# One written list of places for attention, loads and weight pieces in a fused RWKV attention and two-MLP kernel

## The reference

```python
# attention, per batch and head, state is 48 x 48
for t in range(S):
    cur = einsum('bhd,bhe->bhde', u * kt, vt)
    y[t] = einsum('bhd,bhde->bhe', rt, state + cur)
    state = wt[..., None] * state + einsum('bhd,bhe->bhde', kt, vt)
x = y, heads side by side: (2, 768, 384)
# first MLP: 384 -> 1024, taps of 3 along the sequence, gate, -> 384
h = maximum(x @ w_in, 0)
x = (h * sigmoid(conv3(h, conv_w))) @ w_out
# second MLP: layer norm with g_ln, 384 -> 1536 -> 384, added to x
out = x + maximum(norm(x) * g_ln @ w_ch1, 0) @ w_ch2
```

## Time and profile before

| | |
|---|---|
| median of 3 runs | 433.77 us (432.04 to 434.29) |
| profiled execution | 434.07 us |
| its span, first to last instruction | 432.3 us |
| mean granted TensorE clock | 0.944 of full speed |
| TensorE busy | 373.3 us (86%) |
| VectorE busy | 243.1 us (56%) |
| ScalarE busy | 148.4 us (34%) |
| POOL busy | 87.3 us (20%) |

### The profile page before, as it was taken

How to read it: one execution, slowest core, us unless ns; L and a number is a source line. 1 busy time by engine, 2 the same in 40 slices (tenths; PEclk the granted TensorE clock), 3 DMA queues, 4 the chain that set the end, 5 groups by cost and what they waited for, 6 DMA issues and landing times.

```text
span 432.3 us, 8651 instructions
## 1 busy us (share of the span) xinstructions
PE 373.3 (86%) x3255; PEld 352.0 (81%) x3255; DVE 243.1 (56%) x498; ACT 148.4 (34%) x359; POOL 87.3 (20%) x150
## 2 busy tenths in 40 slices
PE   6669796779998499999789999699989699995995
PEld 5558695779998498999689998599988599994994
DVE  4565697795367773368763188862287721385120
ACT  1213384252256221256311256311256211463111
POOL 5344212240220411141032050032050000010001
PEclk9669989698999889999999999989999989998799
DMA  8489131556010133001321010301000000010001
GB/s 140 111 167 199 45 111 55 127 138 152 8 38 1 38 55 58 0 20 36 56 57 20 2 36 20 57 0 22 0 27 12 2 2 2 0 39 0 2 0 36
DMA packets 62786, 20.42 MB, mean 47 GB/s; under 512 B 56959, under 2 KB 61210, under 8 KB 62746
## 3 DMA queue, kind: packets, MB, share of 16 engines
q1 hardware_dynamic: 61520, 19.47, 20.5%
q10 hardware_dynamic: 1226, 0.41, 0.5%
HBM read 17.51 MB, written 2.36 MB: 46 GB/s over the span
## 4 chain that ended last, share of the span: by engine, by line
PE 46%; DVE 8%; ACT 4%; issue 3%; POOL 0%; POOLq 0%; DVEq 0%; ACTq 0%
PE hid L392 7%; PE acc L392 7%; PE hid L393 6%; PE hid L394 6%; PE acc L394 6%; PE acc L393 6%; ACT g_hi L638 2%; PE turn L1002 1%; DVE suf L826 1%; PE y_ps L1047 1%; PE y_ps L1055 1%; DVE g_lo L794 1%; DVE stats L927 1%; PE y_ps L1064 1%; PE pair_a L1020 1%
## 5 line engine op out<-in xcount | busy, mean ns | idle before, releaser
L951 DVE SCALAR_TENSOR_TENSOR g_lo<-hid,g_hi 128x256 fp32r<-128x256 f32 x72 | 30.3, 421 | 112.2 <-ACT g_hi L752 112.1
L752 ACT ACTIVATE g_hi<-hid 128x256 fp32r<-128x256 f32 x72 | 27.7, 385 | 157.2 <-PE acc L394 135.1
L392 PE MATMUL hid<-xc_hi,w_hi 128*128 128x256 f32 x216 | 66.7, 309 | 6.6 <-DVE xc_lo L941 4.9
L393 PE MATMUL hid<-xc_lo,w_hi 128*128 128x256 f32 x216 | 63.1, 292 | 0.0
L394 PE MATMUL hid<-xc_hi,w_lo 128*128 128x256 f32 x216 | 63.0, 292 | 0.0
L773 DVE SCALAR_TENSOR_TENSOR cg<-h_all,cols,cg 128x256 f32<-128x256 f32 x96 | 50.5, 526 | 6.0 <-ACT cg L706 5.4
L392 PEld LDWEIGHTS hid<-xc_hi,w_hi 128*128 128x128 f32 x216 | 43.0, 199 | 10.1 <-issue 6.1
L392 PE MATMUL acc<-w_hi,g_hi 128*128 128x384 f32 x144 | 49.0, 340 | 0.0
L394 PE MATMUL acc<-w_hi,g_lo 128*128 128x384 f32 x144 | 49.0, 340 | 0.0
L393 PE MATMUL acc<-w_lo,g_hi 128*128 128x384 f32 x144 | 48.7, 338 | 0.0
L392 PE MATMUL acc<-wout_hi,g_hi 128*128 128x384 f32 x96 | 35.1, 365 | 11.3 <-DVE g_lo L794 6.3
(11 more groups left out here) (143 smaller groups left out, 775.5 us busy)
## 6 DMA issues: line engine op xcount, KB each, us to landing
w_dec<-in_w SPq DMA_DIRECT2D x12, 192.0 KB, 3.8
k_in<-in_k SPq DMA_DIRECT2D x12, 192.0 KB, 4.3
out<-x SPq DMA_DIRECT2D x12, 192.0 KB, 1.9
r_in<-in_r SPq DMA_DIRECT2D x11, 192.0 KB, 4.0
raw<-in_moe_w_ch SPq DMA_DIRECT2D x4, 384.0 KB
v_in<-in_v SPq DMA_DIRECT2D x12, 96.0 KB, 2.7
cg<-in_moe_w_ch SPq DMA_DIRECT2D x3, 384.0 KB
h_all<-in_moe_w_ch SPq DMA_DIRECT2D x3, 384.0 KB
```

What stands on the lines that cost most here:

```text
L392: pe.matmul(out_ps, lh, rh, start=start and i == 0, stop=False)
L393: pe.matmul(out_ps, lh, rl, start=False, stop=False)
L752: act.activation(a_hi[j % 2][:, :], hid[j % 2][:, 0:GP], ACT.Relu)\
L951: dve.scalar_tensor_tensor(out=a_lo[j % 2][:, :], in0=hid[j % 2][:, 0:GP], scalar=0.0, in1=a_hi[j % 2][:, :].bitcast(F32), op0=ALU.max, op ...
```

## The change

One list of places, written by hand, takes the place of the generator for attention, and it holds loads and fetches too:

- FIRST is the opening. All loads of tiles 0 to 2 but v(2) are issued ahead of weights 0 to 2; six pieces of weights are made before the first hidden, the first of them behind x(1). The rest of the lists (GATING, NORM, TURN, SECOND_MLP) says per group which items follow which place. Hidden waits per j for its half of w_in: three pieces for j < 4, whose pieces now come by halves of the columns. w_in has its rows in plain order.
- A tile's work is cut finer: "scan1" (L811, L816) and "scan2" (the rest), "mid" (`k_mid` and `r_mid` together), "mask", "bonus", "state", "ruk", "middle" (v's middle columns to `v_mid`, POOL) are items of their own.
- k is transposed into `pair_a` and r into `pair_b`, and these wait for the mask of the tile before, not for `turn`; only w and ke use `turn`. In the opening kv uses `hid[1]`.
- `scores` and `bv` are doubled. The two score buffers serve as staging slots 4 and 5 from y(2) on. Pieces 4 to 13 go to `raw`, `x2` and the score buffers, from 14 on to `cg`, `h_all` and `raw`. All low parts are VectorE's.
- x windows: two instead of three; POOL writes the zero edges per tile.
- v comes in one load with the heads side by side, kv as eight matmuls (64 rows of output, 48 columns) instead of four, `bv` in one POOL operation instead of two.

In group 0's second MLP the list has tiles 3 and 4 whole, and tile 5 up to its mask. Between norm(g) and turn(g) stand w(3) | w(6), x(5) | w(9), x(7) | w(11), x(9) | x(11); behind turn(2) and turn(3) stand y(8) and y(10).

```diff
-    WSLOTS = SEQ // G
+    WSLOTS = 2
...
+                 *(t[:, :, :, :].rearrange("p a e s -> p (a e s)")[:, 0:PIECE] for t in scores)]
+        RAW, TWICE, LENT = 3, (1, 2), (4, 5)
...
-        EARLY, MIDDLE = 8, ch1 + half + 1
-        SLOT = ([i % NST for i in range(EARLY)] + [(0, NST - 1)[i % 2] for i in range(MIDDLE - EARLY)]
-                + [1 + i % (NST - 1) for i in range(NP - MIDDLE)])
-        ON_POOL = (1, 3, 5, *range(EARLY, ch1))
+        SECOND = ch1 + half + 1
+        SLOT = [1, 2, 3, 0, 3, 0, 4, 5, 3, 0, 4, 5, 3, 4] + [1 + i % 3 for i in range(NP - SECOND)]
+        ON_POOL = ()
...
-            last = {"in": N_IN - 1, "out": N_IN + j // 2,
+            last = {"in": (N_IN // 2 if j < JF // 2 else N_IN) - 1, "out": N_IN + j // 2,
...
+        FIRST = [("load_w", 0), ("load_k", 0), ("load_v", 0), ("load_w", 1), ("load_k", 1), ("load_r", 1),
+                 ("load_v", 1), ("w", 0), ("k", 0), ("r", 0), ("load_w", 2), ("ruk", 0), ("load_k", 2), ("load_r", 2),
+                 ("fetch", 0), ("fetch", 1), ("fetch", 2), ("middle", 0),
+                 ("scan1", 0), ("scan2", 0), ("w", 1), ("mid", 0), ("sc", 0), ("cols", 0), ("ke", 0),
+                 ("bonus", 0), ("scan1", 1), ("mask", 0), ("kv", 0), ("k", 1), ("r", 1), ("ruk", 1), ("scan2", 1),
+                 ("y", 0), ("w", 2), ("mid", 1), ("sc", 1), ("state", 0), ("x", 0), ("load_v", 2),
+                 ("middle", 1), ("fetch", 3), ("ke", 1), ("bonus", 1), ("scan1", 2), ("mask", 1), ("k", 2), ("r", 2),
+                 ("ruk", 2), ("kv", 1), ("scan2", 2), ("y", 1), ("middle", 2), ("state", 1), ("mid", 2), ("sc", 2),
+                 ("bonus", 2), ("x", 1), ("weights", 0), ("mask", 2), ("weights", 1), ("weights", 2), ("y", 2),
+                 ("weights", 3), ("x", 2), ("fetch", 4), ("fetch", 5), ("fetch", 6), ("fetch", 7),
+                 ("weights", 4), ("weights", 5),
+                 ("fetch", 8), ("fetch", 9), ("load_w", 3), ("load_k", 3), ("load_r", 3), ("load_v", 3)]
...
+        GATING[0] = {0: [("weights", 6), ("fetch", 10)], 1: [("weights", 7), ("fetch", 11)],
+                     2: [("weights", 8), ("fetch", 12)], 3: [("weights", 9), ("fetch", 13)],
+                     5: [("weights", 10), ("fetch", 16)],
+                     7: [("weights", 11)], 8: [("weights", 12), ("k", 3)], 9: [("r", 3), ("weights", 13)]}
+        NORM[0] = [("w", 3)]
+        TURN[0] = [("scan1", 3), ("fetch", 14), ("fetch", 15), ("load_w", 4), ("load_k", 4), ("load_r", 4), ("load_v", 4)]
+        SECOND_MLP[0] = {0: [("ke", 2), ("weights", 14), ("fetch", 17)],
+                         1: [("scan2", 3), ("ruk", 3), ("kv", 2), ("weights", 15), ("fetch", 18)],
+                         2: [("mid", 3), ("weights", 16), ("fetch", 19), ("middle", 3)],
+                         3: [("state", 2), ("w", 4), ("weights", 17), ("fetch", 20)],
+                         4: [("sc", 3), ("weights", 18), ("fetch", 21), ("load_w", 5)],
+                         5: [("bonus", 3), ("mask", 3), ("scan1", 4), ("ke", 3), ("load_k", 5), ("load_r", 5)],
+                         6: [("k", 4), ("r", 4), ("kv", 3), ("weights", 19), ("scan2", 4), ("ruk", 4), ("w", 5)],
+                         7: [("state", 3), ("y", 3), ("mid", 4), ("load_v", 5), ("middle", 4)],
+                         8: [("weights", 20), ("sc", 4), ("x", 3)],
+                         9: [("bonus", 4), ("mask", 4), ("ke", 4), ("scan1", 5)],
+                         10: [("weights", 21), ("y", 4), ("middle", 5), ("k", 5), ("r", 5), ("scan2", 5), ("ruk", 5)],
+                         11: [("x", 4), ("kv", 4), ("mid", 5), ("state", 4), ("load_w", 6), ("load_k", 6), ("load_r", 6)],
+                         12: [("sc", 5)], 13: [("bonus", 5), ("mask", 5), ("load_v", 6)]}
...
+            GATING[g] = {8: made_of(("y", a), ("middle", b)), 9: made_of(("k", c), ("r", c))}
+            NORM[g] = made_of(("w", c), ("x", a))
+            TURN[g] = made_of(("y", b), ("scan1", c), ("load_v", c), ("load_w", d), ("load_k", d), ("load_r", d))
...
         def turn_of(item):
 
-            own_bank = {"w": acc[1], "r": hid[1], "ke": hid[0]}
-            return own_bank.get(item[0], turn) if item in AT_FIRST else turn
+            if item[0] in ("k", "r"):
+                return {"k": pair_a, "r": pair_b}[item[0]]
+            return acc[1] if item[0] == "w" and item in AT_FIRST else turn
...
+                    if n and kind != "w":
+                        pe.wait_ge(s_sc, 2 * n - (kind == "k"))
```

More of the change, by code:

```diff
@@ L93, in rwkv_mlp_kernel @@
         k_mid = sb("k_mid", [P, PAIRS, P])
-        scores = sb("scores", [P, PAIRS, 2, P])
+        scores = [sb(f"scores{b}", [P, PAIRS, 2, P]) for b in range(2)]
         kt_mid = sb("kt_mid", [P, PAIRS, P])
@@ L265, in needed @@
-        def needed(g):
-            return G * (g + 1) + ((g + 1) % WSLOTS > 0)
-        def order():
[L270 to L279, removed]
+        def needed(g):
+            return G * (g + 1) + ((g + 1) % (SEQ // G) > 0)
@@ L292, in first_block @@
                         yield "add", g - 1, j - 4
[L293 to L300, removed]
+                    yield from GATING[g].get(j, [])
             yield from first_block(0, range(3))
@@ L304, in order @@
                 more = g + 1 < GROUPS
-                yield from first_block(g, range(3, JF + 3), {JF: 1, JF + 1: 1})
+                yield from first_block(g, range(3, JF + 3))
                 yield "norm", g
-                yield from some(2)
+                yield from NORM[g]
                 yield "turn", g
-                yield from some(2 if len(parts) > 2 else 0)
+                yield from TURN[g]
                 for j in range(J2):
-                    if g == 0 and (i := next(ahead, None)) is not None:
-                        yield "weights", i
                     yield "hidden2", g, j
@@ L320, in order @@
                     yield "project2", g, J2 - 2 + j
+                    yield from SECOND_MLP[g].get(J2 + j, [])
                 yield "result", g
@@ L397, in halos @@
         def halos(tiles):
-            return sum(2 for n in range(tiles) if (n % G == 0) * n % SEQ or (n % G) and (n + 1) % SEQ)
+            return 2 * tiles
         def by_half(t, at):
@@ L721, in _ @@
                     else:
-                        for which, count in lows(NP - SLOT[::-1].index(0)):
+                        for which, count in emptied(0):
                             act.wait_ge(which, count)
@@ L740, in _ @@
                     else:
-                        for which, count in lows(NP):
+                        for which, count in emptied(RAW):
                             act.wait_ge(which, count)
@@ L1059, in _ @@
-                    pe.wait_ge(s_sc, 2 * (n + 1))
-                    pe.wait_ge(s_ends, n + 2)
-                    for a in range(2):
-                        for q in range(4):
-                            h = 4 * a + q
-                            pe.matmul(y_ps[32 * q:32 * q + 32, a * P:(a + 1) * P],
-                                      by_pair(v_in[b])[:, h // 2, 64 * (h % 2):64 * (h % 2) + 32], scores[:, h // 2, h % 2, :],
-                                      start=False, stop=False, skip_group_check=True)
+                        for i in range(HD // 32):
+                            pe.matmul(rows_32(i), state[n % 2][0:ROW1, i // 3, 32 * (i % 3):32 * (i % 3) + 32],
+                                      r_mid[n % 2][0:ROW1, i // 3, :], start=False, stop=False,
+                                      skip_group_check=True)
```

291 lines of the change are left out of this document (143 added, 148 removed).

## The result

The changed kernel takes 407.94 us, the median of 4 executions (403.80 to 411.47), where the kernel before took 433.75 beside it. The direction was right.

The account below looks back on a forecast made before the run. TensorE was taken as the engine with the most work, so only its waits could shrink, with VectorE's chain setting the new opening. The terms summed to −13.6 us, from 434.1 to 420.5, range 414 to 425.

Parts of the forecast that it names:

- The opening: Up to the first MLP matmul: loads no longer set the end, VectorE's chain does; 42.0 us, a gain of 6.1.
- my placing of items: Opening: items placed one after another in each in-order queue, first MLP matmul at 40.2 us, before 1.8 for half clock.
- The first gating: Group 0's gating: first relu later for pieces 4 and 5, +1.1; more low parts on VectorE, +2.0.
- TensorE's own work: Whole kernel: kv as eight matmuls and y's blocks in another order, same number of instructions: 0, ±0.2 a tile.
- the three new waits: Second MLP of group 0: TensorE waits for a_lo(2) 0.9, state before y(3) 1.7, decays of tile 5 1.5: +4.1.
- Group 1 with its gating: Second normalisation without the wait on k_mid, −2.6; gating gains 0.5, as y(5) lies in front of a wait.
- Group 2: Third normalisation: k_mid wait gone, −0.6; y behind the turn fills the low part's wait, clock stays up, −2.2.
- The clock at turns: Granted clock near 0.5 after turns 0, 1, 4 and 5, and no fall after turns 2 and 3.
- The opening at 38 us with the clock up at turns 0 and 1: Rival, chance 0.10: opening goes as planned, no clock fall at normalisations 0 and 1: 411.5 us.
- Late pieces: Rival, chance 0.08, slower: ScalarE meets pieces 17 to 21 unhidden at 3.0 us each plus clock: 439.9 us.
- VectorE as the bound of all of group 0: Rival, chance 0.17: gating +4.8 in place of 2.0, second MLP +8 in place of 4.1: 427.2 us.
- no change: Rival, chance 0.03: opening gains nothing as loads land late, group 0 takes the upper bounds: 432.2 us at most.

Follow-up runs that it names:

- the last kernel above: Changed kernel with identity matmuls filling the normalisations' gaps, x(4) one place up and more fill in the first gating: 399.11 us, ratio 0.923 to the kernel before.
- the second execution: The changed kernel run once more without edits, on the chip of the follow-up runs: 408.94 us, ratio 0.944 to the kernel before.
- the fillings: Changed kernel with unread identity matmuls before the turns, and behind them where no y stands: 404.08 us, ratio 0.931 to the kernel before.

## Why the prediction was wrong, step by step

**The opening: the term that failed.** I had −6.1 and it is −10.2, 4.1 us of the 10.8 between the forecast and the profiled execution. The price of the slow clock was right: 1.7 us against 1.8 forecast, and the same opening with a full clock, in the last kernel above, is 1.6 us shorter. What was mis-sized is my placing of items, which came to 40.2 us without it, where that kernel shows 36.3. I put the decays of tile 1 at 11 us, four warm-ups behind them, the scores' end at 15.5 and the first mask at 17.0. TensorE turned the decays at 9.95, before the mids were there, and the scores ran from 12.0 to 13.1, right behind r_mid; the mask stands at 14.13, the second at 23.0 and not 27.5, and the last x_lo at 36.9 and not 39.7. Of the gain, the runs name a part: three pieces' parts in the two in-order queues cost 5.5 us even at places later than those of before, the order of the loads nothing, and waiting for six pieces would put the first MLP matmul 2.7 us later. ScalarE's 11.5 us of waits for the loads of the first three pieces before are seen in the trace, and not tested.

**The first gating.** +3.1 forecast, +1.1 measured. ScalarE's two pieces were in place in time for a first relu at 39.6, less than 2 us behind the first matmul. VectorE had 20.6 us of work and not 23.2, though it had two low parts of w_in more than I had counted: I had added the new lows to its 18.4 us and left the rest as it was, but with POOL idle its products and the low parts of the gate took 0.42 us each, not 0.55 and 0.58. The slow clock alone grew by 1.3 us (3.0 in place of 1.7), as much as the whole stage, so TensorE's pace is part of the limit; how far VectorE is, no run tells, as the one that moved lows to POOL gave VectorE more to do.

**TensorE's own work.** I priced kv and the order of the scores at nothing, and took work to be the same. It fell by 5.1 us, and that is on the path where TensorE is busy 58 of 62 us, as in group 2. By kind, with each duration up to the next matmul's start and taken times the granted clock, kv and the scores fell from 16.4 to 14.0 us, most of it by their forms; hidden2's matmuls from 80.0 to 77.2; the transposes of ke from 4.0 to 2.8; the turn's transposes grew by 0.9. The kernel before with new banks has 324.6 us, all of the old work, so the banks aren't the cause. Nor, for hidden2, are the places of attention between the matmuls: in group 5, where neither kernel has any, hidden2's matmuls start 118 to 120 ns apart before and 113 to 114 after. Why the same instructions take less stays open.

**Idle and slow time behind the opening.** −7.5 forecast, −9.1 measured, so near the sum, though not in each part. The waits at the turns were forecast as 2.27 − 0.45 and 1.48 us, and are 1.80 to 1.84 and 1.35 to 1.48. Turn 0 and the second MLP of group 0: −1.7 forecast (with +4.1 for new waits there), −3.5 measured. Of the three new waits one came, 1.60 us before y(3), and another in their stead, 1.60 us of kv(4) for x_lo: 3.2 in place of 4.1. The slow clock was 1.7 us there and not 2.5. Group 1 with its gating: −3.1 against −1.2; the second execution has −2.5, the clock having kept up. Group 2: −2.8 with the wait before its normalisation, against +0.4, since the clock fell at its turn for 1.7 us, which I had excluded. Group 3: −3.7 (its own terms, 5.0 + 1.9 − 3.0, make it −3.9) and −4.2. Group 4: +0.7 and −0.9. Group 5: 0 and −1.2.

Together: 420.5 − 4.1 − 5.1 − 1.6 is 409.7, the profiled execution.

**The clock at turns.** I had it as settled by place: down after turns 0, 1, 4 and 5, up after 2 and 3. The runs show turns 0, 4 and 5 slow in each unfilled profile of the list, turns 1, 2 and 3 slow in one and not in the next. The Trainium skill (TensorE: Matmul & The Clock Gate, section HAM oscillation) has each long gap paid again. Turns 0, 4 and 5 and the fillings, worth 5 us at the turns, agree, though the gaps of 1.8 and 1.5 us here are shorter than those of the page's kernel; turns 1 to 3 show that it isn't so in every execution. The same page (Part 1) calls the gate's effect variable from run to run, and 1.00 against 0.50 behind the same waits agrees.

**The rivals.** The opening at 38 us with the clock up at turns 0 and 1 gave 411.5, the nearest number; it was right on the opening's end, but in the unfilled profiles the clock stayed up at turn 1 only now and then, and at turn 0 never. Late pieces, VectorE as the bound of all of group 0, and no change didn't come about. The range was too narrow below, as no row of it stood for TensorE's work getting less, and only one rival for a better opening.

## What to carry to other kernels

Work that isn't due yet but stands in an in-order queue costs its duration and also its own wait; put weight pieces behind the chain that sets the first output, and only as many as the first user needs. A bank for each user doesn't by itself remove a wait for an engine whose queue is late: the banks alone won 7 us here, but the two long waits at turns only got another name; with VectorE's order changed as well the wait moved to the scores, and the gain was 1 us. The full list, opening and all, won 25. A helper engine can slow the one it helps: four lows on POOL left VectorE with more to do. If a normalisation leaves TensorE gaps of 1.5 to 2 us in a row, put real work there, or else matmuls without use: with them at the normalisations it took 404.1 us and not 408.9, and 399.1 with x(4) moved and two more places filled.

## What the hardware showed that I had not expected

Two gaps of 1.83 and 1.48 us, 0.5 us of work between them, were followed by 5 us at a granted clock of 0.50 in one execution and of 1.00 in another of the same kernel; with them filled, the spread of six executions is as before (4.2 us), and only the last kernel has 2.0. The same matmuls of 256 columns start 118 to 120 ns apart in group 5 of the kernel before and 113 to 114 ns apart in the changed one, with no attention beside them in either. And taking 7.4 us of identity matmuls out of the 38 us opening left its granted clock at 0.95.
